# Strided sparse attention and a rational MLP on one core: smaller cast pieces, later constants, smaller groups of small matmuls, and a new planner for the order

## The reference

```python
scores = q @ k.T / sqrt(64)                       # per batch and head, 576 x 576
mask_local   = (rel >= 0) & (rel < 32)            # heads 0..3
mask_strided = (rel >= 0) & (pos % 32 equal)      # heads 4..7
attn = softmax(where(mask, scores, -1e9)) @ v
x = attn as [4608, 512]
h = x @ w_in                                      # 512 x 2048
P = a0 + a1*h + a2*h^2 + a3*h^3
Q = 1 + |b0|*|h| + |b1|*h^2
out = (P / (Q + 1e-6)) @ w_out                    # 2048 x 512
```

## Time and profile before

| | |
|---|---|
| time, median of 3 runs | 442.07 us (437.69 to 448.58) |
| the profiled execution: time, span | 433.67 us, 431.8 us |
| busy: PE / DVE / ACT / POOL | 342.1 / 321.6 / 311.5 / 70.6 us |
| chain that ended last, by engine | ACT 36%, PE 34%, DVE 11%, DMA 9%, issue 8% |

### The profile page before, as it was taken

How to read it: one execution, slowest core, us unless ns; L and a number is a source line. 1 busy time by engine, 2 the same in 40 slices (tenths; PEclk the granted TensorE clock), 3 DMA queues, 4 the chain that set the end, 5 groups by cost and what they waited for, 6 DMA issues and landing times.

```text
span 431.8 us, 10538 instructions
## 1 busy us (share of the span) xinstructions
PE 342.1 (79%) x4770; PEld 163.1 (38%) x4770; DVE 321.6 (74%) x255; ACT 311.5 (72%) x340; POOL 70.6 (16%) x104
## 2 busy tenths in 40 slices
PE   1475878975991598989968978699799999967685
PEld 0343435432441244444423533344444433423232
DVE  1252778875984449798884797758898998898991
ACT  2121856492972479797939795759979999999972
POOL 8554000070053008005301220000000000000000
PEclk9999989986996699889989999899979999997989
DMA  7999990899989969997998799945032111010012
GB/s 110 143 218 142 227 132 10 196 142 127 192 174 129 176 149 200 150 209 143 145 185 162 162 134 209 142 56 133 26 80 56 49 49 51 7 41 26 24 49 97
DMA packets 117116, 52.35 MB, mean 121 GB/s; under 512 B 96464, under 2 KB 110032, under 8 KB 116688
## 3 DMA queue, kind: packets, MB, share of 16 engines
q0 software_dynamic: 30656, 18.37, 41.2%
q1 hardware_dynamic: 86416, 33.32, 41.1%
HBM read 36.87 MB, written 20.25 MB: 132 GB/s over the span
## 4 chain that ended last, share of the span: by engine, by line
ACT 36%; PE 34%; DVE 11%; DMA 9%; issue 8%; SPq 1%; ACTq 0%
PE ps L952 13%; PE ps L884 12%; ACT u L917 10%; ACT u L922 8%; ACT h L888 7%; ACT z L904 7%; DMA xt<-xs 4%; DMA ptS<-pS 3%; ACT os L960 3%; DVE u L913 2%; DMA coef<-in_moe_b_dram 2%; DVE u L911 1%; DVE z L928 1%; PE ps L774 1%; PE ps L665 1%
## 5 line engine op out<-in xcount | busy, mean ns | idle before, releaser
L952 PE MATMUL ps<-Wout,h 128*128 128x512 bf16 x576 | 146.7, 397 | 17.5 <-DVE h L936 6.9
L884 PE MATMUL ps<-xt,Win 128*128 128x512 bf16 x576 | 148.2, 399 | 11.3 <-DMA xt<-xs 4.8
L888 ACT ACTIVATE h<-ps 128x512 bf16<-128x512 f32 x144 | 80.8, 622 | 44.2 <-PE ps L884 44.1
L952 PEld LDWEIGHTS ps<-Wout,h 128*128 128x128 bf16 x576 | 56.1, 101 | 88.2 <-issue 15.7
L884 PEld LDWEIGHTS ps<-xt,Win 128*128 128x128 bf16 x576 | 54.6, 101 | 83.2 <-issue 17.0
L917 ACT ACTIVATE u<-u,consts 128x2048 bf16<-128x2048 bf16 (+1 forms) x40 | 71.4, 1839 | 2.3 <-DVE u L913 2.2
L922 ACT ACTIVATE u<-u 128x2048 bf16<-128x2048 bf16 (+1 forms) x40 | 68.1, 1747 | 0.1
L904 ACT ACTIVATE z<-h 128x2048 bf16<-128x2048 bf16 (+1 forms) x34 | 60.4, 1832 | 1.9 <-DVE h L936 1.7
L936 DVE TENSOR_TENSOR h<-z,u 128x4096 bf16<-128x4096 bf16 (+2 forms) x21 | 41.6, 1983 | 6.7 <-ACT u L922 6.3
L928 DVE TENSOR_TENSOR z<-z,h 128x4096 bf16<-128x4096 bf16 (+2 forms) x21 | 41.6, 1979 | 0.5
L932 DVE TENSOR_TENSOR z<-z,h 128x4096 bf16<-128x4096 bf16 (+2 forms) x21 | 41.5, 1976 | 0.5
(11 more groups left out here) (70 smaller groups left out, 213.0 us busy)
## 6 DMA issues: line engine op xcount, KB each, us to landing
out_dram<-os SPq DMA_DIRECT2D x36, 256.0 KB, 2.4
qk<-in_q_dram POOLq DMA_DIRECT2D x12, 288.0 KB, 6.8
qk<-in_k_dram POOLq DMA_DIRECT2D x12, 288.0 KB, 8.9
vL<-in_v_dram POOLq DMA_DIRECT2D x32, 72.0 KB, 11.3
vS<-in_v_dram POOLq DMA_DIRECT2D x32, 72.0 KB, 11.6
vL<-vL SPq DMA_DIRECT2D x16, 138.1 KB, 2.6
Win<-in_moe_w_in_dram POOLq DMA_DIRECT2D x2, 1024.0 KB, 18.7
Wout<-in_moe_w_out_dram POOLq DMA_DIRECT2D x2, 1024.0 KB, 27.1
```

The costliest lines, as they stand in the source:

```text
L884: r = e.matmul(bank(ph, 0, CH), Win[:, kk, f * 128:(f + 1) * 128], xt.t[:, kk, :], start=(kk == 0), stop=(kk == NK1 - 1))
L888: P.op("act", lambda e, f=f, ph=ph, h=h, f0=f0: e.activation(h.t[:, f - f0, :], bank(ph, 0, CH), AF.Copy), 0.6, ky, r=[ph], w=[h], occ=0.48)
L952: r = e.matmul(bank(po, 0, Fout), h.t[:, j, m * 128:(m + 1) * 128], Wout[:, kk, :], start=(kk == 0), stop=(kk == NF - 1))
```

## The change

1. `bulk` splits each cast of q or k for batches 2 to 7 into rows of 256 elements (512 B written) where it had 16 pieces of 9216 elements.
2. The identity alone is loaded first; MS, BO and M0 become `T_m`, loaded after the first q has landed; the coefficients come after the last k of batch 0. The 1 + 1e-6 constant becomes a DVE memset.
3. `weights_in` loads W_in in four pieces with tiles of their own in place of two.
4. Score and v-product groups are handed to the planner 16 (or 20) matmuls at a time.
5. 98 matmuls of 2 columns run at the very start (`tiny`).
6. The planner counts PE's instructions (two per matmul) in lines of 256 and a time at which the next line is there, holds back an operation that would stall if another is ready, slows PE after a stretch in which it was little used, and shares the DMA engines between the queues by packet time. Durations and DMA figures are new.
7. Every operation gets a tag, and `OFF` (a table of numbers, cut here to a few entries) adds a fixed number to the key of each tag. Batch 1's loads have their key 21 later (`LK1`).

Sizes of the MLP groups, buffers, the engine of each operation and all arithmetic stay.

```diff
+LINE, LINE0 = 256, 62
+OFF = {
+    "G0": -45, "G1": -94.7, "G2": -151.6, ...
+    "L0": 84.8, "L1": -190.2, ... "V1": -87.2, ... "c1": 90.3, "c2": 158, ...
+    "l2": 58.9, ... "m0.0": -129.6, ... "z8.2": -232.4, "z8.3": -114.8,
+}
...
+        self.slow_line, self.fast_line, self.look = 6.0, 3.4, 30.0
...
+    def op(self, eng, maker, dur, key, r=(), w=(), m=(), dma=None, occ=None, after=(), hard=(), mm=0):
...
+        o.key += OFF.get(self.tag, 0.0)
...
+    def reach(self, o, t):
...
+        while c + n - f > LINE:
+            f += LINE - c
+            x = t + stall + dur * f / n
+            if x < ok:
+                stall += ok - x
+                x = ok
+            c = 0
+            ok = x + (self.slow_line if self.dq["sw"] else self.fast_line)
...
+                ph, ps = cur["hw"][3], cur["sw"][3]
+                both = max(ph, ps) + 0.3 * min(ph, ps)
+                rate = {"hw": ph / both, "sw": ps / both}
...
-    for i, (dst, arr) in enumerate(((IDN, np.eye(128, dtype=np.float32)), (MS, ms), (M0, m0), (BO, bo))):
+    const(0, IDN, np.eye(128, dtype=np.float32), T_c)
+    P.op("dve", lambda e: e.memset(eps1, float(np.float32(1.0 + 1e-6))), 0.1, -9.6e5, w=[T_k])
+    def late_consts(first, last):
+        for i, (dst, arr) in enumerate(((MS, ms), (BO, bo), (M0, m0))):
+            const(i + 1, dst, arr, T_m, after=first)
...
+    def tiny(e):
+        r = None
+        for i in range(98):
+            r = e.matmul(bank(TD, 0, 2, 0, 2), warm[:, 0:2], warm[:, 0:2], start=True, stop=True, skip_group_check=True)
+        return r
+    P.op("pe", tiny, 3.5, -9e5, r=[T_w], w=[TD], mm=98)
...
-            n = HL * S * D // 16
+            n = HL * S * D
             P.op("pool", lambda e: e.dma_start(
-                bass.AP(tensor=d_t, offset=off, ap=[[n, 16], [1, n]]),
-                bass.AP(tensor=s_t.tensor, offset=s_t.offset + (b * H + h0) * S * D, ap=[[n, 16], [1, n]])),
-                1.1, key, w=[t], dma=(1.4, 2.0), after=after)
+                bass.AP(tensor=d_t, offset=off, ap=[[256, n // 256], [1, 256]]),
+                bass.AP(tensor=s_t.tensor, offset=s_t.offset + (b * H + h0) * S * D, ap=[[256, n // 256], [1, 256]])),
+                0.65, key, w=[t], dma=(2.1, 2.4, 0.058), after=after)
...
-        w = Fmid // 2
+        w = Fmid // 4
...
-        for h0 in (0, 2):
-            P.op("pe", lambda e, h0=h0: sscore(e, (h0, h0 + 1)), 64 * 0.014, key, r=[T_c, sqk], m=[SS])
+        for h in range(HL):
+            for b0 in (0, 2):
+                P.op("pe", lambda e, h=h, b0=b0: sscore(e, h, (b0, b0 + 1)), 16 * 0.014, key, r=[sqk], m=[SS], mm=16)
...
-        P.op("pe", lambda e: lscore(e, range(4)), 64 * 0.013, key, r=[lqt, lkt], m=[SL])
+        for g in range(4):
+            P.op("pe", lambda e, g=g: lscore(e, (g,)), 16 * 0.013, key, r=[lqt, lkt], m=[SL], mm=16)
...
+    LK1 = 33
     vS = {0: casts(0, -100)}
+    late_consts(stage[0, "qs"].w, stage[0, "kl"].w)
     st = loads(0, -50, vS[0])
-    weights_in(0, -90)
-    weights_in(1, -89)
+    for i in range(4):
+        weights_in(i, -90 + i)
...
-            st = loads(b + 1, key + 12, vS[b + 1])
+            st = loads(b + 1, key + (LK1 if b == 0 else 12), vS[b + 1])
```

More of the change, by code:

```diff
@@ L122, in _place, with flow, done @@
         return best
+    def reach(self, o, t):
+        w = int(t / WIN)
+        k = 1.0
+        if self.wbusy.get(w - 1, 0.0) < 0.5 * WIN:
+            k = 2.0 if o.dur > 0.1 * o.mm else 1.3
+        dur = o.dur * k
+        n, stall = 2 * o.mm, 0.0
+        c, ok = self.icnt, self.lineok
+        f = 0
+        while c + n - f > LINE:
[6 more added lines that the diff above has]
+            ok = x + (self.slow_line if self.dq["sw"] else self.fast_line)
+        return stall, dur - o.dur + stall, dur, (c + n - f, ok)
+    def flow(self, t):
+        while self.dnow < t:
+            now = self.dnow
+            cur = {}
+            nxt = t
+            for q in ("hw", "sw"):
+                if self.dq[q]:
+                    j = self.dq[q][0]
+                    if j[0] <= now + 1e-9:
+                        cur[q] = j
+                    else:
+                        nxt = min(nxt, j[0])
+            rate = {q: 1.0 for q in cur}
+            if len(cur) == 2:
+                ph, ps = cur["hw"][3], cur["sw"][3]
+                both = max(ph, ps) + 0.3 * min(ph, ps)
+                rate = {"hw": ph / both, "sw": ps / both}
+            for q, j in cur.items():
+                nxt = min(nxt, now + j[1] / rate[q])
+            self.dnow = nxt
+            end = False
+            for q, j in cur.items():
+                j[1] -= (nxt - now) * rate[q]
+                if j[1] <= 1e-9:
+                    self.dq[q].pop(0)
+                    self.done(j[2], nxt + 0.5 * j[2].dma[1])
+                    end = True
+            if end:
+                return True
+        return False
+    def done(self, o, fin):
+        o.fin = fin
+        for b in o.banks:
+            b.left -= 1
+            if b.left == 0:
+                f = max(x.fin for x in b.ops) + 0.1
+                for i in range(b.at, b.at + b.n):
+                    self.blast[i] = list(b.ops)
+                    self.bfree[i] = f
+        for u in o.users:
+            lat = (0.15 if o in u.hard else 0.035) if u.eng == o.eng and o.dma is None else 0.1
+            u.ready = max(u.ready, o.fin + lat)
+            u.ndep -= 1
+            if u.ndep == 0:
+                self.rq[u.eng].append(u)
     def schedule(self):
@@ L128, in schedule @@
             o.ready = 0.0
+        for o in self.ops:
             for d in o.deps:
@@ L167, in schedule @@
                         soon = (s, o)
+                if held is not None and pick is None:
+                    pick = held[:2]
                 c = pick or soon
@@ L170, in schedule @@
                     best = (c[0], e, c[1])
-            assert best is not None, "no bank"
+            if best is None:
+                assert self.flow(1e6), "no bank"
+                continue
             t, e, o = best
+            if self.flow(t):
+                continue
             if o.bank is not None:
@@ L182, in schedule @@
             ready[e].remove(o)
-            free[e] = t + o.occ
-            o.start = t
[L185 to L198, removed]
+            dur, occ = o.dur, o.occ
+            if e == "pe":
+                st, more, busy, (self.icnt, self.lineok) = self.reach(o, t)
+                dur, occ = dur + more, occ + more
+                w = int((t + st) / WIN)
+                x = min(busy, (w + 1) * WIN - t - st)
+                self.wbusy[w] = self.wbusy.get(w, 0.0) + x
+                self.wbusy[w + 1] = self.wbusy.get(w + 1, 0.0) + busy - x
+            free[e] = t + occ
+            o.start = t
             order[e].append(o)
             left -= 1
[L201 to L214, removed]
+            if o.dma is not None:
+                self.dq["sw" if e == "pool" else "hw"].append([t + dur + 0.5 * o.dma[1], o.dma[0], o, o.dma[2]])
+            else:
+                self.done(o, t + dur)
+        while any(self.dq.values()):
+            self.flow(1e6)
         self.order = order
@@ L348, in bass_strided_sparse_attn__then__act_rational_pade_kernel @@
     Wout = sb("Wout", [128, NF, Fout])
-    T_win = [Tile(f"win{i}") for i in range(2)]
+    T_win = [Tile(f"win{i}") for i in range(4)]
     T_wout = [Tile(f"wout{i}") for i in range(2)]
@@ L716, in attention @@
         t0 = b * S
+        P.tag = f"V{b}"
         key += 8
@@ L732, in attention, with sav @@
             AS = Banks(2)
-            def sav(e, AS=AS, b2=b2):
+            def sav(e, g0, AS=AS, b2=b2):
                 r = None
-                for g in range(8):
+                for g in (g0, g0 + 1):
                     p, h = divmod(g, 4)
@@ L746, in sav @@
                 return r
-            P.op("pe", sav, 64 * 0.014, key, r=[ptS, vS], w=[AS])
+            for g0 in range(0, 8, 2):
+                P.op("pe", lambda e, g0=g0, sav=sav: sav(e, g0), 16 * 0.014, key, r=[ptS, vS],
+                     **(dict(m=[AS]) if g0 else dict(w=[AS])), mm=16)
             P.op("dve", lambda e, AS=AS, b2=b2: e.tensor_tensor(
@@ L778, in lav @@
             r = None
-            for g in range(5):
+            for g in gs:
                 for pair in range(2):
```

151 lines of the change are left out of this document (93 added, 58 removed), and 20 rows, old and new, of the table OFF.

## The result

The changed kernel took 422.27 us (median of 4 runs, 420.97 to 429.32), the kernel before on the same chip 443.95 (437.69 to 448.58): ratio 0.959 [0.946, 0.972], faster. The profiled execution took 421.34 us (span 419.5), 12.3 us less than the profiled one of before. The forecast of 416 us lies 6 us beside the measured time; how its terms fared is another matter. Some executions of most kernels are 1 to 5% longer at a lower granted clock: ratios in this document leave them out and medians do not, so in e9 and e10 the two don't match, and of e2, e3 and e4, whose profiled executions were such, only packets, places and what stands on the chain are read from the trace.

What follows compares the result with a forecast made beforehand. No engine was full; holes in ACT's work before 300 us were taken to bound the kernel. Terms -13 + 2 - 5 - 6 - 4 = -26 gave 407.7 us, times 1.0194 is 416; forecast 398 to 425, wider range 394 to 438.

Steps and rivals of the forecast that it cites:

- sum of -26 us: Whole kernel: the five terms -13, +2, -5, -6 and -4 added, from the profiled 433.7 us to 407.7.
- factor 1.0194: Whole kernel: multiplies the summed profiled time, since the median 442.07 us was 1.9% above the profiled execution; gives 415.6.
- Bound: Whole kernel: no engine is full; ACT idles 120 us, mostly before 300 us, and the change is worth the holes it closes.
- Cast pieces, what they free: Transposing DMAs behind POOL's casts: smaller pieces let them land sooner, 4 us at 91.97 and 9 at 126.82; -13 (0 to -24).
- the rivals: Four other outcomes: waits change place 0.22, it gains more 0.13, transfers become the bound 0.08, fetch gains nothing 0.05.
- Cast pieces, what they cost: Casts from batch 2 on: more DMA time, +2.3 us per batch of four; on the path +2 (0 to +32).
- third rival: DMA engines, batches 2 to 7: transfers become the bound, 76 ns a piece, 5.3 us a batch; 459 us scaled; chance 0.08.
- Start: First 40 us: later coefficients gain 1 us, one of two instruction stalls goes for 4; -5 (0 to -9).
- Later stalls: PE's four later instruction stalls, 12.64 us: groups of 16 let other work hide the fetch, half counted; -6 (0 to -12.6).
- fourth rival: PE's instruction fetch: crossing a block is mostly hidden, so this part gains nothing; -16, 426 us scaled; chance 0.05.
- The order: All five queues: landing times nearer the true ones cut waits such as SP's at the xS stores; -4 (-16 to +16).
- first rival: All queues: waits change place, engines stand at the next late thing; -10, 432 us scaled, range 425 to 442; chance 0.22.

Runs made afterwards that it cites:

- e9: Changed kernel, masks sent right behind the identity, |b| later on DVE, casts not waiting for v's copy, v loads of batches 3 to 6 after the previous P transpose: 0.9497.
- e10: Changed kernel with 2 tiny matmuls at the start in place of 98, orders unchanged: 433.89 us, 0.9761 of the kernel before.
- e2: Kernel before with only real 512 B pieces in its casts, same queues and order: 440.06 us, 0.9976 of the kernel before.
- e3: Changed kernel with MS, BO and M0 sent right behind the identity, other queues unchanged: 420.33 us, 0.9566 of the kernel before.
- e4: Changed kernel with the table of offsets emptied, groups of 16 and model of instruction lots kept: 0.9804 of the kernel before.
- e1: Changed kernel with cast rows interleaved so that neighbours don't touch, giving real 512 B pieces: 423.75 us, 0.9684 of the kernel before.
- e5: Changed kernel without most of the q and k casts of batches 3 to 7 (16 of 576 rows stay): 403.67 us, 0.9161 of the kernel before.
- e6: Changed kernel without 17 of 18 parts of vL's load in batches 3 to 7, casts whole: 410.14 us, 0.9352 of the kernel before.
- e11: Kernel before with its old planner, only the score and v products planned in groups of 16 matmuls: 1.0045 of the kernel before.
- e12: Changed kernel without offsets and with score and v products in groups of 64 and 36 again, model of lots kept: 0.9617 of the kernel before.

## Why the prediction was right, and where it was not

The range and the sign were right. The size came out near by luck, by two errors that partly cancel: the sum of -26 us was -12.3 on the profiled execution (433.67 to 421.34), 13.7 us too much, and the factor 1.0194 from there to the median is 1.002 in the changed kernel (422.27 / 421.34), 7 us the other way.

*Bound.* Right in the main: ACT has the same work, and while the span fell by 12.3 us, ACT's idle time (span less busy) fell by 11.4, from 120.3 to 108.9. The forecast that it would fall before 160 us, from 77 to 55, failed: it is 75.2 there.

*Cast pieces, what they free: -13.* The step that failed, twice. The change cuts no pieces, which none of the rivals foresaw. And cut pieces free nothing (e1, e2). "While such a piece is under way its engine seems to do nothing for the other queue" was read from long landings behind four casts, and the loads of v were overlooked: in the kernel before they follow the casts at once, around the transpose of 91.97 us.

```profile
89.60 3.47 POOL L462 DMA_DIRECT2D vL<-in_v_dram  x4
91.97 1.92 SPq L571 DMA_TRANSPOSE ptS<-pS  x1
93.06 2.34 POOL L469 DMA_DIRECT2D vS<-in_v_dram  x4
```

The longest landing of a P transpose there, 13.2 us, belongs to one issued at 124.86 us, when only two of the four casts beside it had been issued, so traffic issued later seems to delay it too. The amount of traffic around the transpose explains these landings with any piece size, and e5 and e6 bear it out for both kinds. PE's waits for transfers fell by 1.5 us instead of 13. The wait for xt did leave the chain; as the pieces are the same, that is the order's doing. The Trainium skill (DMA: Bandwidth & Descriptors, Queues, rings and completion order) has a rule that fits e1: an engine changes between queues after a packet, which there means a bundle of several descriptors, not after each, so that 36 small pieces in place of one need not give a transpose 36 turns. No run here shows the turns themselves.

*Cast pieces, what they cost: +2 (0 to +32).* Nothing in the changed kernel, as nothing is cut. In e1 the landings grew by 0.4 and 0.9 us a cast, which is about the 0.6 us that the sum took (2.3 for four) and hardly leaves the spread of kernels with 18 KB pieces; e1 stands 0.9% above the changed kernel, with intervals that overlap. The third rival's 5.3 us a batch did not come. The overhead of small DMAs cited with it (the Trainium skill, Perfetto Trace Analysis, DMA Optimizations) is not clear of that spread in any run here.

*Start: -5 (0 to -9).* It was +3.3, outside the bounds. The coefficients no longer hold DVE's first copy (at 7.07 us, before at 12.20), but two errors ate more than that: MS, BO and M0 were costed "at nothing, covered by the loads of k", but they land at 18.00 (8.29 + 9.71) and PE stood 4.9 us for them; and the tiny matmuls were to take one of the two stalls away, but both stay (2.95 + 4.86 = 7.81 us, before 3.75 + 3.94 = 7.69). The bound of 8.56 us for lost cover was stated and not taken into the sum's range.

*Later stalls: -6 (0 to -12.6).* The stalls fell by the size forecast: "issue" is 5.2 us less over PE's waits, and on the chain 7.1% of the span instead of 8.4%, 29.8 us for 36.3. Where four stood on the chain behind the start with 12.64 us, one of 5.53 is left of over 2.2 us. That the kernel is shorter for it isn't shown: groups of 16 alone take off 4.5 us of stalls (e11), as the prediction's way has it, and the time stays. Its fourth rival, a fetch that is mostly hidden (the Trainium skill, Runtime: NRT & Kernel Launch, Instruction fetch mechanics), is not borne out as to the stalls: 16.9 us of them are in the changed kernel's trace. As to time, e11 speaks for that rival.

*The order: -4 (-16 to +16).* Mis-sized. Waits for DVE and ACT fell by 11.6 us, the loads' wait behind xS went from 24.1 us at worst to 15.1, and against e4 the offsets are worth 2.2%, some 9 us, though e12 is as fast without them.

```profile
SPq L881 <- DVE xS L873: 21.3, 3, 15.1
```

So the first rival, waits that change place, describes the transfers, though the time came out better than its 425 to 442, and the order carries most of what was won.

## What to carry over

When a change makes transfers smaller, count the packets by size before and after: rows of 512 B that touch each other in memory moved here as pieces of 18 KB, whatever the pattern said. A transposing DMA that is late beside other traffic here was late by that traffic's amount, not by its piece size. Moving the traffic freed it (e9), but the gain was nearly lost to other waits and instruction stalls; what an order drawn for the new times would keep wasn't tried. Where a planner's order is what changes, cost it by what each queue waits for, and take a spread of some 2% for the draw. A stall's length in one trace is weak evidence: the same one took 4.86 and 7.60 us.

## What was not expected of the hardware

A cast of 288 KB between two places in DRAM moves as 16 packets of 18 KB when its rows adjoin, whether the pattern names rows of 9216 elements or of 256 (384 such packets in 24 casts), and as 576 packets of 512 B to 2 KB when its neighbours in the pattern lie apart (13824 in 24 casts); its median landing in e1 is 0.4 to 0.9 us later, hardly outside the spread. A DMA transpose that lands in 3.0 us at its shortest took up to 18.5 beside casts and loads of v with pieces of 18 KB, and up to 14.1 with 512 B (e1). With 96 tiny matmuls fewer at the start, whose results nobody reads, PE's four first long stalls come 32 matmuls earlier in an unchanged order, which fits lots of 128 matmuls.
